# Choosing the experts' slots of a routed mixture: 16 of 24 tiles during the last dense group, the table in fp32r

## The reference, cut to what matters

```python
def _moe_ref(x, w_gate, w1, w2):             # N, D, E, F = 3072, 384, 8, 1024
    ...                                      # P: 8 Sinkhorn iterations on exp(x @ w_gate)
    for e in range(E):
        h = np.maximum(x @ w1[e], 0.0)
        out += P[:, e:e + 1] * (h @ w2[e])

def _moe2_ref(x, expert_emb, tau, w1, w2):
    xn = x / (norm(x) + 1e-06)
    en = expert_emb / (norm(expert_emb) + 1e-06)
    logits = xn @ en.T / tau
    expert_idx = np.argmax(logits, axis=1)
    probs = softmax(logits)                  # shifted by the row's maximum, sum + 1e-9
    gate_w = probs[np.arange(N), expert_idx]
    for e in range(E):
        mask = expert_idx == e
        h = np.maximum(x[mask] @ w1[e], 0.0)
        out[mask] = gate_w[mask, None] * (h @ w2[e])
```

## Time and profile before

| | |
|---|---|
| median of 3 runs | 2337.61 us (2337.05 to 2340.84) |
| the profiled execution | 2338.97 us, its span 2337.1 us |
| PE busy | 2217.1 us, 95% |
| PEld busy | 2053.0 us, 88% |
| DVE busy | 1011.3 us, 43% |
| ACT busy | 600.6 us, 26% |
| POOL busy | 95.6 us, 4% |
| mean granted TensorE clock | 0.964 |
| chain that ended last | PE 88%, DVE 5%, DMA 3%, SP's queue 2% |

### The profile page before, as it was taken

The page is one execution under the profiler, slowest core; times in us unless marked ns, Lnnn a source line. Parts: engine busy times, 40 slices in busy tenths (PEclk is TensorE's granted clock), DMA queues, the critical chain, the costliest instruction groups (busy, mean ns, idle before and its releaser), DMA issues.

```text
span 2337.1 us, 42563 instructions
## 1 busy us (share of the span) xinstructions
PE 2217.1 (95%) x17911; PEld 2053.0 (88%) x17911; DVE 1011.3 (43%) x1853; ACT 600.6 (26%) x1014; POOL 95.6 (4%) x92
## 2 busy tenths in 40 slices
PE   4789999999999999999999999999999998599998
PEld 4788898988999998999899899989999888599998
DVE  7575465345332333333233233332323223667764
ACT  2232232331111111111111111111111112366664
POOL 0000000000000000000000000000000000122221
PEclk8699999999999999999999999999999998699999
DMA  8644434331000000000000000000000011576662
GB/s 279 181 135 133 132 113 121 97 129 55 1 28 1 28 25 4 27 1 27 1 28 27 1 28 1 27 1 28 1 1 1 14 28 41 182 247 234 233 242 72
DMA packets 152488, 172.65 MB, mean 74 GB/s; under 512 B 81564, under 2 KB 112448, under 8 KB 152322
## 3 DMA queue, kind: packets, MB, share of 16 engines
q1 hardware_dynamic: 145186, 158.92, 21.1%
q0 software_dynamic: 3968, 10.82, 1.3%
q10 hardware_dynamic: 3168, 0.39, 0.1%
HBM read 144.15 MB, written 27.33 MB: 73 GB/s over the span
## 4 chain that ended last, share of the span: by engine, by line
PE 88%; DVE 5%; DMA 3%; SPq 2%; issue 1%; ACT 1%; POOL 0%; POOLq 0%; ACTq 0%; DVEq 0%
PE psA L1571 22%; PE psH L1586 15%; PE psB L1571 8%; PE psB L1586 7%; PE psY L1586 7%; PE psY L1682 5%; PE psH L1468 4%; PE psA L1352 4%; PE psY L1483 3%; PE psA L1668 3%; PE psB L1668 3%; PE psB L1441 1%; PE psB L1451 1%; SPq L414 1%; DVE products L983 1%
## 5 line engine op out<-in xcount | busy, mean ns | idle before, releaser
L1571 PE MATMUL psA<-X,wh 128*128 128x512 f32 x1440 | 456.0, 398 | 6.4 <-DVE wl L1132 4.1
L1139 DVE SCALAR_TENSOR_TENSOR hl<-psA,hh 128x512 fp32r<-128x512 f32 x240 | 166.0, 692 | 648.3 <-ACT hh L792 648.2
L792 ACT ACTIVATE hh<-psA 128x512 fp32r<-128x512 f32 x240 | 143.8, 599 | 855.8 <-PE psA L1571 855.8
L1571 PEld LDWEIGHTS psA<-X,wh 128*128 128x128 f32 x1440 | 271.0, 191 | 53.5 <-issue 7.9
L1571 PE MATMUL psA<-X,wl 128*128 128x512 f32 x720 | 288.2, 400 | 0.0
L1586 PE MATMUL psH<-wh,hh 128*128 128x384 f32 x672 | 228.7, 340 | 0.0
L1586 PE MATMUL psH<-wh,hl 128*128 128x384 f32 x672 | 227.4, 338 | 0.0
L1586 PE MATMUL psH<-wl,hh 128*128 128x384 f32 x672 | 226.0, 336 | 0.0
L1139 DVE SCALAR_TENSOR_TENSOR hl<-psB,hh 128x512 fp32r<-128x512 f32 x96 | 66.5, 693 | 277.6 <-ACT hh L792 277.6
L1571 PE MATMUL psB<-X,wh 128*128 128x512 f32 x576 | 179.2, 392 | 0.0
L1301 DVE TENSOR_TENSOR vl<-vs,vh 128x768 fp32r<-128x768 f32 x152 | 145.7, 961 | 56.8 <-ACT vh L829 55.9
(11 more groups left out here) (255 smaller groups left out, 4117.4 us busy)
## 6 DMA issues: line engine op xcount, KB each, us to landing
vs<-v_d SPq DMA_DIRECT2D x38, 768.0 KB
vs<-v_d SPq DMA_DIRECT2D x19, 1536.0 KB, 11.8
ws<-w_d SPq DMA_DIRECT2D x28, 768.0 KB, 6.0
kT<-kT_d SPq DMA_DIRECT2D x17, 512.0 KB, 4.3
qT<-qT_d SPq DMA_DIRECT2D x15, 512.0 KB, 5.0
a_scratch<-an SPq DMA_DIRECT2D x12, 512.0 KB, 3.4
kq<-kn_d SPq DMA_DIRECT2D x6, 768.0 KB, 6.5
vn<-vn_d SPq DMA_DIRECT2D x12, 384.0 KB, 4.0
```

Of the source, the lines that this page charges most:

```text
L792: act.activation(hh[kk % 3][:, :], ps_h[kk % (2 if last else 3)], ACT.Relu).then_inc(hh_ready, 1)
L1139: dve.scalar_tensor_tensor(hl[b][:, :], ps_h[bank], 0.0, hh[b][:, :].bitcast(F32), ALU.max, ALU.subtract).then_inc(hl_ready, 1)
L1571: mm = pe.matmul(to, a[half][:, c, col], X[:, 2 * g:2 * g + 2, b, c, :], start=(n == 0), stop=(n == 3 * KC - 1))
```

## The change

- **Turns spread.** `route` is gone. `turn(t)` (three transposes) and `logits(t)` stand singly between `hidden` and `give`: turns in the second and third step of a group, logits in the third and fourth. DVE's `take` stands before and after `low_hidden`. The last four tiles, after the last `give`, have four PSUM banks and four `x2T`, and ACT copies two of them.
- **Scale.** 1/tau goes into the embeddings (`enT`), and the one-hot is taken from unnormalised logits; the norms are used for the gates alone, later.
- **16 tiles early.** `choose(0)`, `prefixes(0)` and `ranks(0)` run on DVE in the last three steps for tiles 0 to 15, `counts(0)` on PE in the step before the last. The same functions with 1 do the other 8 tiles after the last `give`. `oh`, `ones` and `before` are fp32r.
- **Offsets.** The two doubling sums over experts become a product with a constant 8 by 8 triangle and a reduction. Place and step come from a token's rank among its expert's tokens by a mask and a shift; single tiles have the first seven columns of the table.
- **Table.** fp32r, in two tables: token numbers as two digits to the base 64, and, later, gates as a high and a low part. `at_tile` and `entry` are made in three rounds of 8 tiles, `at_place` in six of 4, of which two come before the offsets. DVE makes `eid` after the entries, then `who`, then the norms' part, gates and `entry_g`.
- **Order at the first slot.** PE: first table, `features(0)`, second table, slot 0. DVE and ACT: pieces 0 and 1, `features(0)`, then pieces 2 to 7; DVE reads the second table before piece 2, and ACT waits for the gates before piece 4.

```diff
@@ constants
-PLACED = 6
+PLACED = 4
+TABBED = 8
+BASE = 64
+NTA = 4 * GT
+FIRST = 2
@@ GpSimd
-                pool.wait_ge(acc_done, NALL)
+                pool.wait_ge(l1_done, STEPS * (E - 2) + STEPS // 2 + 1)
                 pool.memset(zrow[:, :], 0.0).then_inc(rt_zero, 1)
-                pool.memset(ones[:, :], 1.0).then_inc(rt_ones, 1)
@@ ScalarE, after the last dense step
+                squares(NT - 4)
+                squares(NT - 3)
+                take(NT - 4)
+                take(NT - 2)
+                squares(NT - 2)
+                squares(NT - 1)
@@ ScalarE, first slot
-                for f in range(KF // 2, KF):
-                    if f == KF // 2 + 2:
+                for f in range(KF):
+                    if f == FIRST:
                         features(0, 0, False)
+                    if f == KF // 2:
+                        act.wait_ge(gates_ready, 1)
                     split_piece(0, 0, 0, f)
@@ VectorE, expert(e, last)
+                        done = GT * (g - NGRP - 1)
+                        if last and done >= 0 and f in (2, 3):
+                            take(done + 2 * f - 3)
                         low_hidden(STEPS * (e - 1) + kk, kk % 3, kk % (2 if last else 3))
...
-                        if last and kk >= STEPS // 2 + FB and kk % FB == 2:
-                            take(kk // FB - NGRP - 1)
+                        if last and done >= 0 and f in (1, 2):
+                            take(done + 2 * f - 2)
...
+                        if last and kk == STEPS - 3:
+                            choose(0)
+                        if last and kk == STEPS - 2:
+                            prefixes(0)
+                        if last and kk == STEPS - 1:
+                            ranks(0)
                     add(e, 1, NGRP - 1)
                     if last:
-                        take(NGRP - 1)
+                        take(NT - 3)
+                        take(NT - 1)
+                def choose(m):
+                    q, n = tiles_of(m)
+                    dve.wait_ge(lg_done, m + 1)
+                    dve.tensor_copy(picked[:, q, :], sc_x2[:, q, :]).then_inc(picked_ready, 1)
+                    dve.wait_ge(picked_ready, m + 1)
+                    chain(rt, dve.tensor_reduce(mxs[:, q], picked[:, q, :], AX.X, ALU.max))
+                    chain(rt, dve.tensor_tensor(raw[:, q, :], picked[:, q, :], rows_of(mxs[:, q], n), ALU.is_equal))
...
+                    dve.tensor_tensor(oh[:, q, :], raw[:, q, :], rows_of(first[:, q], n), ALU.is_equal).then_inc(oh_ready, 1)
+                places(0)
+                choose(1)
+                places(PLACED)
+                prefixes(1)
...
+                for i in range(2):
+                    dve.tensor_tensor(grown[:, i, :, :], own[:, i, :].unsqueeze(1).to_broadcast([P, E, E]), smaller, ALU.mult).then_inc(rt, 1)
...
+                chain(rt, dve.tensor_reduce(excl[:, :, :], grown[:, :, :, :], AX.X, ALU.add))
...
+                ranks(1)
...
+                for t in range(0, NT, TABBED):
+                    q = slice(t, t + TABBED)
+                    for u in range(t, t + TABBED, PLACED):
+                        if u >= 2 * PLACED:
+                            places(u)
+                    chain(rt, dve.tensor_tensor(at_tile[:, q, :], ...))
+                    dve.tensor_tensor(entry[:, q, :, :], ...).then_inc(entry_ready, 1)
...
+                dve.wait_ge(tab_done, 1)
+                chain(rt, dve.tensor_scalar(whof[:, :], ps_tab[0][:, 0:NTAB], float(BASE), float(N), ALU.mult, ALU.add))
+                dve.tensor_tensor(who[:, :], whof[:, :], ps_tab[0][:, NTAB:2 * NTAB], ALU.add).then_inc(who_ready, 1)
@@ VectorE, first slot
-                for f in range(KF // 2, KF):
-                    if f == KF // 2 + 2:
+                for f in range(KF):
+                    if f == FIRST:
                         features(0, 0, False)
+                        dve.wait_ge(tab_g_done, 1)
+                        dve.tensor_copy(gates[:, :], ps_tab[1][:, 0:NTAB]).then_inc(rt, 1)
+                        dve.wait_ge(rt, count[0] + 1)
+                        dve.tensor_tensor(gates[:, :], gates[:, :], ps_tab[1][:, NTAB:2 * NTAB], ALU.add).then_inc(gates_ready, 1)
                     split_piece(0, 0, f)
@@ TensorE
+                def turn(t):
+                    tail = t >= NT - 4
+                    pe.wait_ge(acc_done, NALL - NT + t + 1)
+                    if t >= 1 and not tail or t == NT - 4:
+                        pe.wait_ge(tr_ready, t)
+                    for k in range(KC):
+                        mm = pe.transpose(ps_x2[t % 4 if tail else 0][:, k, :], acc[:, t, k * P:(k + 1) * P], ident)
+                    mm.then_inc(tr_done, 1)
...
                 for kk in range(1, STEPS):
                     hidden(E - 1, kk)
+                    f, done = kk % FB, GT * (kk // FB - NGRP - 1)
+                    if done >= 0:
+                        if f in (2, 3):
+                            logits(done + 2 * f - 4)
+                            logits(done + 2 * f - 3)
+                        if f in (1, 2):
+                            turn(done + 2 * f - 2)
+                    if kk == STEPS - 2:
+                        counts(0)
                     give(E - 1, kk - 1)
-                    if kk >= STEPS // 2 + FB and kk % FB == 2:
-                        route(kk // FB - NGRP - 1)
+                    if done >= 0 and f in (1, 2):
+                        turn(done + 2 * f - 1)
                 give(E - 1, STEPS - 1)
-                route(NGRP - 1)
+                for t in range(NT - 4, NT):
+                    turn(t)
+                for t in range(NT - 4, NT):
+                    logits(t)
+                counts(1)
...
+                table(entry, entry_ready, ps_tab[0]).then_inc(tab_done, 1)
...
                 features(0, 0, False, ST)
+                table(entry_g, entry_g_ready, ps_tab[1]).then_inc(tab_g_done, 1)
```

More of the change, by code:

```diff
@@ L229, in build @@
-        cu = [keep(f"cu{i}", [P, NT, E]) for i in range(2)]
-        cs = [keep(f"cs{i}", [P, 2, E]) for i in range(3)]
+        lg, ex = (keep(n, [P, NT, E]) for n in ("lg", "ex"))
+        cnt, grown = keep("cnt", [P, E, MAXS]), keep("grown", [P, 2, E, E])
+        own, excl, incl = (keep(n, [P, 2, E]) for n in ("own", "excl", "incl"))
+        start, twice, last, gap = (keep(n, [P, E]) for n in ("start", "twice", "last", "gap"))
+        wrap = keep("wrap", [P, 1])
         thr, es = keep("thr", [P, NSLOT]), keep("es", [P, NSLOT])
-        mxs, gate, posf = (keep(n, [P, NT]) for n in ("mxs", "gate", "posf"))
@@ L233, in build @@
-        ones = keep("ones", [P, P])
-        cnt = keep("cnt", [P, E, MAXS])
+        gate, gate2 = keep("gate", [P, NT]), keep("gate2", [P, NT, 2], F32R)
         se, ef = keep("se", [P, NSLOT, E]), keep("ef", [P, NSLOT])
[L236 to L239, removed]
+        tilef, over_end = keep("tilef", [P, NT]), keep("over_end", [P, NT])
@@ new lines, in _ @@
+                dve.tensor_scalar(twice[:, :], own[:, 0, :], float(ST), None, ALU.mult).then_inc(rt, 1)
+                dve.scalar_tensor_tensor(wrap[:, :], excl[:, 1, E - 1:E], float(-NTAB), own[:, 1, E - 1:E], ALU.add, ALU.add).then_inc(rt, 1)
+                count[0] += 4
+                dve.wait_ge(rt, count[0])
+                dve.tensor_tensor(last[:, :], last[:, :], excl[:, 1, :], ALU.add).then_inc(rt, 1)
+                dve.tensor_tensor(gap[:, :], twice[:, :], start[:, :], ALU.add).then_inc(rt, 1)
@@ new lines, in _ @@
+                count[0] += 2
+                dve.wait_ge(rt, count[0])
+                chain(rt, dve.tensor_tensor(gap[:, :], last[:, :], gap[:, :], ALU.subtract))
+                ranks(1)
+                step = part_f[:, 1, :]
+                chain(rt, dve.tensor_tensor(spare[:, :, :], rows_of(step), cols_of(twice[:, :]), ALU.is_ge))
+                chain(rt, dve.tensor_tensor(spare[:, :, :], spare[:, :, :], cols_of(gap[:, :]), ALU.mult))
+                chain(rt, dve.tensor_tensor(spare[:, :, :], spare[:, :, :], cols_of(start[:, :]), ALU.add))
@@ L1253, in _ @@
+                chain(rt, dve.tensor_tensor(incl[:, :, :], excl[:, :, :], own[:, :, :], ALU.add))
+                dve.scalar_tensor_tensor(thr[:, :], made["small"], incl[:, 1, E - 1:E], made["slots"], ALU.mult, ALU.add).then_inc(rt, 1)
+                dve.tensor_scalar(incl[:, 0, :], incl[:, 0, :], float(ST), None, ALU.mult).then_inc(rt, 1)
+                count[0] += 2
                 chain(rt, dve.tensor_tensor(se[:, :, :], incl[:, 1, :].unsqueeze(1).to_broadcast([P, NSLOT, E]),
@@ new lines, in _ @@
+                chain(rt, dve.reciprocal(gate[:, :], rank[:, :]))
+                chain(rt, dve.tensor_copy(gate2[:, :, 0], gate[:, :]))
+                chain(rt, dve.tensor_tensor(gate2[:, :, 1], gate[:, :], gate2[:, :, 0].bitcast(F32), ALU.subtract))
+                for t in range(0, NT, TABBED):
+                    q = slice(t, t + TABBED)
```

(2 more changed lines are left out.)

316 lines of the change are left out of this document (160 added, 156 removed).

## The result

The changed kernel took 2310.87 us (median of four runs, 2310.08 to 2317.49), the kernel before 2337.39 (four runs, 2337.05 to 2340.84): ratio 0.989, 95% interval 0.987 to 0.991. The forecast was 2316.5, in a range of 2309 to 2326.

A forecast was written before the change was run, and what follows sets the result against it. TensorE matmuls bound the kernel (88% of the chain), except in the last dense expert and the gap before the routed experts. Savings 15.7 + 5.4 = 21.1 took 2338.97 to 2317.9 profiled, median 2316.5 us; 8-in-10 range 2309 to 2326.

The forecast's parts named there:

- the logits term: Last dense expert: six logits passes a tile between dense matmuls, taken at 0.75 us for each of 20 tiles.
- Part 1: Last dense expert: turns and logits spread over the steps cost 21.9 us against 37.6 for five routes, 15.7 saved.
- (a): Sign in the last expert: first light work to last give about 95 us in place of 111, clock 1.00 throughout.
- Rivals 2, 3 and 4: Last expert: clock falls each group (2325, chance 0.14); clock stays low (2388, 0.04); late DVE copies, no gain (0.02).
- The chain to who: Gap after the last dense give: who ready at +24.25 us from that give's end against +39.3, 15.1 early.
- The loaded gather: Gap, first slot: second gather, issued as weights begin to move, takes 7.0 us; features at +33.1, not +29.3.
- Rival 1: Gap: the gathers are not delayed, features at +29.3, first give 3.9 us faster, total 2312.6; chance 0.20.
- The order behind the features: Gap: transposes, then gate table (+40.0), then six DVE splits (+45.9), put the first routed give at +46.5 us.
- (d): Sign in the gap: second table's 24 matmuls behind the transposes, 5.3 us long, VectorE idle for it.
- (e): Sign in the gap: PE idle some 2 us before the first routed give, ended by gl.
- My shares of the 15.1 won on who: Gap: 5.4 us saved; 3.9 go to the loaded gather, 5.3 to the gate table, the rest to six splits.
- From there the routed slots are unchanged.: Routed experts after the first routed give: no change in time was forecast there.

The follow-up runs named there:

- b_spread: The kernel before with only the turns and logits of tiles 0 to 19 spread over the steps: 2319.14 us, ratio 0.993.
- a_who_first: The changed kernel with who made before the eid chain on DVE, so first gathers are issued before any weights: 2317.58 us, ratio 0.991.
- a_gates_first: The changed kernel with the gate table ahead of features(0) on PE, and DVE reading the gates before features(0): 2311.02 us, ratio 0.989.
- a_pieces: The changed kernel with splits 5 to 7 of the first slot's weights moved behind its first low halves: 2311.22 us, ratio 0.989.
- c_after: The changed kernel run again, unedited: 2312.82 us (median of six runs, 2306.33 to 2315.61), ratio 0.990.

## Why the prediction held, and where it was off

The forecast for the profiled execution was 2317.9, 21.1 below the old; it was 2310.28, 28.7 below. Of the 7.6 between them, 4.5 are the scatter of the start and 2.8 the dense part (2.4 of it light work, which is the logits term). The last 0.3 hide two misses: the gap up to the first `give` was 1.7 shorter than forecast, and 1.4 were lost after it, where nothing was forecast. Against the mean of all ten runs, 2312.4, the forecast of 2316.5 is 4.1 too high.

1. *Part 1, forecast 15.7, measured 18.5.* The mechanism is right: there is no DVE wait, the clock is 1.00, and b_spread shows it alone. The figure in (a) is off. It had "about 95" from the first light work, and 99.4 were measured, because (a) left out that the light work now starts 6.3 earlier in the order of steps; from the same place 18.1 are saved. The mis-sized term is "six passes in 0.73 to 0.75": between dense matmuls six cost 0.62, and 20 x 0.13 = 2.6. I had taken the price from a block of six that stood in front of a wait, where the end of the last pass counts, and not from one among dense matmuls, where the next one covers it. The turn at 0.33, from a row of the latter kind, was exact. Rivals 2, 3 and 4 fall: every window of the last expert is at 1.00 and no wait for a copy is left.
2. *The chain to who, forecast +24.25, measured +23.3.* Step by step: logits +4.1 (forecast 4.5), counts +6.3 (6.9), gap +10.5 (11.2), tilef +14.6 (15.35), last entry +20.25 (21.0), table +22.3 (23.1). Of the 0.9, 0.4 is the logits price again (24 passes in 2.59 in the chain, where 3.0 and more were taken), 0.35 lies in the ops up to the gap, 0.2 at the end; from the gap to the last entry the sum was right. fp32r with 62 columns cost what I had taken, 0.22: the second table's 24 took 5.31. Eight alone took 1.89, the end of the last one included.
3. *The loaded gather, forecast 7.0, measured 6.8* from its issue at 1978.91 to the first transpose. Rival 1 falls, and a_who_first shows the cause: with the weights issued later the same gathers landed in 3.4 and 3.0. The page DMA: Bandwidth & Descriptors of the Trainium skill (Queues, rings and completion order) has each DMA engine take turns between queues. The estimate by it (+31, from an issue at +26.15) is 4.85 from issue to landing, 2.0 short of what was measured, and nearer than the 3.1 of an idle queue. The row from inside the loop was right; the features came 1.0 before the forecast because who did.
4. *The order behind the features.* Gate table 5.3 with DVE idle (d), then six splits 5.29, then PE idle 2.11 ended by gl (e): each as forecast. First `give` +44.65 against +46.5, old +51.73: 7.1 sooner, not 5.4. Of the 1.85, 1.0 was there at the features, the rest came in small parts up to the `give`. My shares of the 15.1 won on who (it was 16.0) are shown in part. The 5.3 for the table behind the features was too much: a_gates_first takes back 2.6, a_pieces 2.2 of the splits, both together 3.95. The 3.9 for the loaded gather no run isolates.
5. *"From there the routed slots are unchanged."* True in c_after (308.35 against 308.72), not in the first profile (310.10), where the clock fell once more. This step was stated without a bound, and should have had one of about 2: over the changed kernels the rest is 308.28 to 310.24.

The main error of the sum, the price of the logits from an isolated block, stood in both parts (2.6 and 0.4) and made the forecast timid. Without the scatter of the start and the loss after the first `give`, which it knew nothing of, the saving is 25.6 against its 21.1. Open: what decides whether the clock falls behind the idle 2 us (five profiles have more than 2, four of them a fall), and what makes the first 520 us vary.

## What to carry to other kernels

Take the price of a small group of matmuls from a row where it stands between dense ones; in front of a wait the end of the last one comes on top. When one long wait is cut, draw every other chain that ends at the same instruction before counting the gain: here who came 16 us sooner and the first `give` 7, and features 4.45 sooner, bought with weights 2.6 later, gave nothing. A stage can be measured to some 0.3 us by events of two profiles where the total needs ten runs to show 5.

## What the runs showed of the hardware

- Small fp32 logits matmuls of 8 columns: 1.24 for twelve passes between dense ones at full clock, so 0.62 for six; 0.73 for six as a block in front of a wait, with the end of the last pass in it (the twelve with theirs are 1.40).
- fp32r of 62 columns took 0.22 a matmul at the low clock (5.31 for 24); plain fp32 of the same shape two passes of 0.22 (10.47 for 48). The single fp32r pass costs as much as one of the two. Few columns made nothing cheaper there: passes of 8 columns cost 0.21 (twelve in 2.56), and fp32r matmuls of 256 columns, the first routed `hidden`, also start 0.21 apart (at 1992.67, 1992.88 and 1993.09).
- Gathers of 0.2 MB: 3.0 and 3.4 when no weights had been issued yet (a_who_first), 6.2 in the median while the weights of two slots, 3 MB each, were being loaded (the changed kernel).
- Nearly the same idle time of PE, 2.11 and 2.05, was followed by a fall to 0.50 in one profile of the changed kernel and not in the other. Idle times of 2.43, 2.49 and 5.05 in three others were followed by one, an idle time of 1.40 (a_gates_first) by none. The page TensorE: Matmul & The Clock Gate of the Trainium skill (A second HAM failure mode: psum-queue depth-cycling) describes a clock that goes up and down through short idle times between groups of matmuls. The traces here show a single fall after a single idle time, in four of five profiles.
